# Two-block merges of a triangular inverse crossed over the PE array, their evictions shared by two engines, and the attention steps put in other slots

## The reference, cut to what matters

```
for t in range(768):                       # 4 batches x 8 heads, head_dim 48
    y[t]   = q[t] @ state
    state += beta[t] * outer(k_n[t], v[t] - k_n[t] @ state)      # k_n = k/(|k|+1e-6)
x = y as 3072 tokens x 384
x = leaky_relu(x @ w_in, 0.01) @ w_out     # w_in 384x2048, w_out 2048x384
e = argmax(x @ w_gate + bias[modality]);  out = gate * (relu(x @ w1[e]) @ w2[e])   # 8 experts
```

## Time and profile before

| | |
|---|---|
| median of 3 runs | 987.36 us (984.31 to 990.70) |
| the profiled execution | 978.93 us, of which the span shown by the profile is 977.2 us |
| granted TensorE clock, mean over the span | 0.957 |
| tile n = 3 (`up(3,0)` to `up(4,0)`) | 421.32 to 524.06 us |
| `up(5,0)` begins | 618.30 us |

### The profile page before, as it was taken

How to read it: one execution, slowest core, us unless ns; L and a number is a source line. 1 busy time by engine, 2 the same in 40 slices (tenths; PEclk the granted TensorE clock), 3 DMA queues, 4 the chain that set the end, 5 groups by cost and what they waited for, 6 DMA issues and landing times.

```text
span 977.2 us, 26906 instructions
## 1 busy us (share of the span) xinstructions
PE 870.9 (89%) x10528; PEld 766.0 (78%) x10529; DVE 553.5 (57%) x1578; ACT 350.6 (36%) x609; POOL 87.6 (9%) x100
## 2 busy tenths in 40 slices
PE   3775889989999998999989999999969999999962
PEld 3664678878888887888878888888759898889862
DVE  4974994588638862798359842344642333333350
ACT  3364335542545253444444342323411212121230
POOL 1000000000020002000100001010121212121210
PEclk9965899999999999999999999999999999999996
DMA  9904272345143533344153313255051111111122
GB/s 127 337 4 75 62 150 68 68 107 101 34 92 74 104 62 52 99 86 81 41 102 84 74 28 84 58 94 175 32 171 33 48 32 48 32 48 32 40 74 73
DMA packets 148308, 77.92 MB, mean 80 GB/s; under 512 B 112496, under 2 KB 144240, under 8 KB 147824
## 3 DMA queue, kind: packets, MB, share of 16 engines
q1 hardware_dynamic: 143264, 66.59, 30.4%
q0 software_dynamic: 4096, 9.48, 3.2%
q10 hardware_dynamic: 848, 0.39, 0.2%
HBM read 59.30 MB, written 13.21 MB: 74 GB/s over the span
## 4 chain that ended last, share of the span: by engine, by line
PE 67%; DVE 15%; ACT 7%; DMA 4%; issue 3%; SPq 1%; ACTq 1%; DVEq 0%; POOL 0%; POOLq 0%
PE bank L518 17%; PE bank L503 14%; PE bank L605 11%; PE bank L580 10%; DVE inv_t L1299 2%; DVE inv_tmp L1293 2%; PE bank L590 2%; PE bank L381 2%; PE bank L410 2%; ACT diag L987 2%; DVE g_raw L1368 1%; PE bank L484 1%; DVE tr L1305 1%; PE bank L471 1%; DVE inv_a L1255 1%
## 5 line engine op out<-in xcount | busy, mean ns | idle before, releaser
L518 PE MATMUL bank<-wo_hi,g_hi 128*128 128x392 f32 x384 | 139.1, 362 | 7.3 <-DVE g_lo L1373 4.0
L518 PE MATMUL bank<-wo_hi,g_lo 128*128 128x392 f32 x384 | 132.2, 344 | 0.0
L518 PE MATMUL bank<-wo_lo,g_hi 128*128 128x392 f32 x384 | 132.1, 344 | 0.0
L1368 DVE SCALAR_TENSOR_TENSOR g_raw<-g_raw 128x512 f32<-128x512 f32 x96 | 66.3, 691 | 105.0 <-ACT g_raw L1043 105.0
L503 PE MATMUL bank<-x_hi,wi_hi 128*128 128x512 f32 x288 | 118.3, 411 | 6.2 <-ACT g_raw L1043 3.4
L1043 ACT ACTIVATE g_raw<-bank 128x512 f32<-128x512 f32 x96 | 57.3, 597 | 170.5 <-PE bank L503 170.1
L503 PE MATMUL bank<-x_hi,wi_lo 128*128 128x512 f32 x288 | 114.0, 396 | 0.0
L503 PE MATMUL bank<-x_lo,wi_hi 128*128 128x512 f32 x288 | 113.9, 395 | 0.0
L1050 ACT ACTIVATE g_hi<-g_raw 128x512 fp32r<-128x512 f32 x96 | 60.7, 632 | 116.9 <-DVE g_raw L1368 116.9
L1373 DVE TENSOR_TENSOR g_lo<-g_raw,g_hi 128x512 fp32r<-128x512 f32 x96 | 66.3, 691 | 41.9 <-ACT g_hi L1050 41.7
L518 PEld LDWEIGHTS bank<-wo_hi,g_hi 128*128 128x128 f32 x384 | 72.7, 189 | 13.8 <-issue 6.0
(11 more groups left out here) (215 smaller groups left out, 1493.3 us busy)
## 6 DMA issues: line engine op xcount, KB each, us to landing
wo_lo<-wo_lo_d SPq DMA_DIRECT2D x80, 196.0 KB, 2.4
w_raw<-in_moe_w SPq DMA_DIRECT2D x6, 1536.0 KB, 8.4
x_rows<-stage SPq DMA_DIRECT2D x6, 770.0 KB, 6.2
kq_in_rows<-in_k SPq DMA_DIRECT2D x6, 768.0 KB, 7.0
k_raw<-in_k SPq DMA_DIRECT2D x24, 192.0 KB, 4.0
vals<-in_v SPq DMA_DIRECT2D x48, 96.0 KB, 2.9
kq_in_rows<-in_q SPq DMA_DIRECT2D x6, 768.0 KB, 8.8
x_raw<-y_t SPq DMA_DIRECT2D x33, 96.0 KB, 2.4
```

The source lines that it names most:

```text
L518: mm = pe.matmul(acc[i][:, 0:DX], g[f % 2][:, P * i:P * i + P], w, start=(f == 0 and k == 0), stop=(f == FT - 1 and k == 2))
L1368: dve.scalar_tensor_tensor(out=g_raw[f % 2][:], in0=g_raw[f % 2][:], scalar=0.01, in1=g_raw[f % 2][:], op0=ALU.mult, op1=ALU.max).then_inc ...
```

## The change

- `merge_x` and `merge_p` are crossed: even and odd pairs use different halves of the array's columns and go to different banks (X,0 and X,1 are now even and odd pairs, not the first and the second sixteen groups). Both are moved behind `down` of their slots 5 and 6. `merge_p` waits for both X banks, `updates` for both P banks.
- ACT evicts the odd X bank (behind `copy_diag` in its order), DVE the even one.
- The elimination runs in slots 12 to 4 instead of 13 to 4.
- `scale_v` (values times norm) and `split_x` (`x_lo`) go from DVE to Pool, but for the first tile's `x_lo`.
- `gram_q(.., 1)` goes ahead of `up` in slot 0; `old_values(.., 0)` with its `sub_w` from slot 5 to slot 3; `outputs` from slots 10 and 11 to 11 and 12; `gram_k` from slots 10 and 11 to both sides of `down` in slot 10, with its evictions; `state_sum(.., 1, ..)` and `add_s` from slot 12 to slot 11, `norm` (DVE) and `roots` (ACT) too; `scale_gram` to slot 12.
- SP loads the values one slot earlier (slot 15 instead of 0 of the next tile).

```diff
-INV_AT = {13: (0, 5), 14: (5, 9), 15: (9, 13), 0: (13, 17), 1: (17, 21), 2: (21, 25), 3: (25, 30), 4: (30, INV)}
+INV_AT = {12: (0, 4), 13: (4, 8), 14: (8, 11), 15: (11, 14), 0: (14, 17), 1: (17, 20), 2: (20, 24), 3: (24, 28), 4: (28, INV)}
@@ PE
-            def merge_x(t, m):
+            def merge_x(t):
                 pe.wait_ge(s.tr_ready, t + 1)
-                b, done = fill(("X", t, m))
+                to = [fill(("X", t, odd)) for odd in range(2)]
                 for j in range(16):
-                    for hh in range(2):
-                        mm = pe.matmul(b[low_p(hh), BLK * j:BLK * j + BLK], inv_s[up_p(hh), 16 * m + j, BLK:CH],
-                                       tr[up_p(hh), 16 * m + j, :], start=True, stop=True)
-                mm.then_inc(done, 1)
+                    for odd in range(2):
+                        for hh in range(2):
+                            mm = pe.matmul(to[odd][0][low_p(hh ^ odd), BLK * j:BLK * j + BLK], inv_s[up_p(hh), 2 * j + odd, BLK:CH],
+                                           tr[up_p(hh), 2 * j + odd, :], start=True, stop=True)
+                        if j == 15:
+                            mm.then_inc(to[odd][1], 1)
...
-            def merge_p(t, m):
+            def merge_p(t):
                 pe.wait_ge(s.td_ev, 4 * t + 2)
-                pe.wait_ge(*is_drained(("X", t, m)))
-                b, done = fill(("P", t, m))
+                for odd in range(2):
+                    pe.wait_ge(*is_drained(("X", t, odd)))
+                to = [fill(("P", t, odd)) for odd in range(2)]
...
             def updates(t, c):
                 pe.wait_ge(s.td_ev, 4 * t + 4)
-                pe.wait_ge(*is_drained(("P", t, c)))
+                for odd in range(2):
+                    pe.wait_ge(*is_drained(("P", t, odd)))
...
@@ PE slot, ahead of down
+                if cur and f == 0:
+                    gram_q(n + 1, 1)
                 if ff and f < FT - 1:
                     up(n, f + 1)
...
-                    if f < 3:
+                    if f in (1, 2):
                         gram_q(n + 1, f + 1)
-                    if f == 5:
-                        merge_x(n + 1, 0)
-                        merge_x(n + 1, 1)
-                    if f == 6:
-                        merge_p(n + 1, 0)
-                        merge_p(n + 1, 1)
+                    if f == 3 and n >= 0:
+                        old_values(n + 1, 0)
...
-                    if f == 10:
+                    if f == 10 and n < 0:
                         outputs(n + 1, 0)
-                        if n < 0:
-                            outputs(n + 1, 1)
+                        outputs(n + 1, 1)
                     if f == 11 and n >= 0:
+                        outputs(n + 1, 0)
+                    if f == 12 and n >= 0:
                         outputs(n + 1, 1)
-                    if f == 12:
-                        state_sum(n + 1, 1, 0)
...
                 if nxt:
+                    if f == 10:
+                        gram_k(n + 2, 0)
@@ PE slot, behind down
-                    if f == 5 and n >= 0:
-                        old_values(n + 1, 0)
+                    if f == 5:
+                        merge_x(n + 1)
+                    if f == 6:
+                        merge_p(n + 1)
...
-                    if f == 12:
-                        state_sum(n + 1, 1, 1)
...
                     if f == 10:
-                        gram_k(n + 2, 0)
-                    if f == 11:
                         gram_k(n + 2, 1)
+                if cur and f == 11:
+                    state_sum(n + 1, 1, 0)
+                    state_sum(n + 1, 1, 1)
@@ SP slot
-                if f == 0 and n >= 0 and is_set(n + 1):
-                    sp.wait_ge(*is_filled(("U", n, 1, 1)))
-                    load_values(n + 1)
...
+                if f == 15 and n >= -1 and is_set(n + 2):
+                    sp.wait_ge(*is_filled(("U", n + 1, 1, 1)))
+                    load_values(n + 2)
@@ Pool
-            for t in range(1, SETS):
-                pool.wait_ge(s.tt_ready, t)
-                pool.memset(inv_t[:], 0.0).then_inc(s.tm_zero, 1)
-                if t == 2:
+            def scale_v(t):
+                pool.wait_ge(s.v_in, 128 * t + 128)
+                pool.wait_ge(s.den_rdy, t + 1)
+                pool.tensor_tensor(vals[:], vals[:], den_s[:].unsqueeze(2).broadcast_to([P, GROUPS, HD]), ALU.mult
+                                   ).then_inc(s.vals_rdy, 1)
+
+            def split_x(n):
+                pool.wait_ge(s.xh, n + 1)
+                pool.tensor_tensor(x_lo[:], x_raw[:], x_hi[:].bitcast(F32), ALU.subtract).then_inc(s.x_rdy, 1)
+
+
+            for n in range(-1, TT - 1):
+                scale_v(n + 1)
+                if is_set(n + 2):
+                    pool.wait_ge(s.tt_ready, n + 2)
+                    pool.memset(inv_t[:], 0.0).then_inc(s.tm_zero, 1)
+                if n == 1:
                     pool.wait_ge(s.list_out, 16)
-                if t >= 2:
-                    scatter_ids(t - 2)
+                if n >= 1:
+                    scatter_ids(n - 1)
+                if n >= 0:
+                    split_x(n + 1)
@@ ACT
+            def copy_x(t, odd):
+                act.wait_ge(*is_filled(("X", t, odd)))
+                act.wait_ge(s.tr_ready, t + 1)
+                for hh in range(2):
+                    mm = act.activation(tr[low_p(hh), odd::2, :],
+                                        att_bank(("X", t, odd))[low_p(hh ^ odd), :].rearrange("p (g t) -> p g t", g=16), ACT.Copy, scale=-1.0)
+                mm.then_inc(drain(("X", t, odd)), 1)
...
                     if f == 5:
                         copy_diag(n + 1)
+                        copy_x(n + 1, 1)
...
                     if f == 10:
                         copy_gram(n + 2, 0, 0)
+                        copy_gram(n + 2, 1, 0)
                     if f == 11:
-                        copy_gram(n + 2, 1, 0)
-                    if f == 12:
                         if n == -1:
                             split_x(0)
                         roots(n + 2)
@@ DVE slot
-                if nxt and f == 13:
+                if nxt and f == 12:
                     scale_gram(n + 2)
...
-                if 0 <= n < TT - 1 and f == 14:
-                    split_x(n + 1)
                 if cur:
+                    if f == 3 and n >= 0:
+                        sub_w(n + 1, 0, 0)
+                        sub_w(n + 1, 0, 1)
                     if f == 5:
-                        copy_x(n + 1, 1)
-                        scale_v(n + 1)
-                        if n >= 0:
-                            sub_w(n + 1, 0, 0)
-                            sub_w(n + 1, 0, 1)
+                        copy_x(n + 1, 0)
...
-                if nxt:
-                    if f == 10:
-                        copy_gram(n + 2, 0, 1)
-                    if f == 11:
-                        copy_gram(n + 2, 1, 1)
-                    if f == 12:
-                        if n == -1:
-                            split_x(0)
-                        norm(n + 2)
-                if cur and f == 12:
+                if nxt and f == 10:
+                    copy_gram(n + 2, 0, 1)
+                    copy_gram(n + 2, 1, 1)
+                if cur and f == 11:
                     add_s(n + 1, 1, 0)
                     add_s(n + 1, 1, 1)
+                if n == -1 and f == 11:
+                    split_first_x()
+                if nxt and f == 11:
+                    norm(n + 2)
```

67 lines of the change are left out of this document (29 added, 38 removed).

## The result

Both kernels were timed in turn on the same chip: before 987.45 us (984.31 to 990.7), after **1023.64 us** (1022.33 to 1029.37), four runs each; the ratio is 1.0377, with a 95% interval of 1.0326 to 1.0429. I had said 992, at most 1007. The profiled spans are 977.2 and 1021.1 us, so 43.9 us have to be found. PE's busy time grew by 7.4 us against the earlier trace rows, although the merges are shorter; the rest is waiting. Part of both is the clock: between `up(0, 0)` and `up(5, 0)` it stands at 0.50 for 63.6 us of the trace, against 15.6 before; half the pace for 48 us more is up to 24 us (an estimate).

A forecast was written before the change was run, and what follows sets the result against it. The attention tiles were taken as bound by PE (busy 89%). Terms: n = -1 and 0 +3.8, n = 1 to 3 +1.5, n = 4 +2.1, fetch wait -2.1; in all +5 us, giving 992 us, 8 in 10 from 977 to 1007.

The forecast's parts named there:

- The merges halve: merge_x and merge_p: crossing takes half off each merge of 2.14 us, 1.07 us less each.
- The waits of 0.69 and 1.1 us: PE's waits ahead of up(1) (0.69 us) and of merge_x behind tr (1.09 us), both said to go.
- that at `queries_t`: PE's wait of 1.26 us ahead of queries_t, said to go since add_s comes before norm.
- ACT's queue holds `merge_p`: merge_p: PE waits 2.35 us for ACT's copy_x(1), queued behind copy_diag, where it waited nowhere.
- the bank of the fourth KK product: Slot 10: the fourth product waits 1.0 us for the first one's bank, which ACT drains by copy_gram.
- e + 14.35: e is the end of up(6); copy_p was put ready at e + 14.45, PE at e + 13.35: 1.1 us wait at updates.
- x_lo on Pool: Ahead of up(n+1, 0): Pool's x_lo takes 2.9 us; PE waits 0.9 us in n = 0 to 3, 1.8 in n = 4.
- my slower rival: x_lo of 4.35 us or more on Pool holds up each tile and the clock falls: 16 us, 1008; chance 0.18.
- The clock at merge_p: Behind the 2.35 us wait at merge_p the clock falls to half; +0.8 us a tile, bounds 0 and 1.7.
- -2.1 - 1.1 + 2.35 + 1.1 + 0.8: up(6) to up(9): merges halved, merge_x wait gone, waits added at merge_p and updates, slower clock.
- The fetch stops: PE's 2.49 us wait for its own instructions in outputs of n = 2; half of 2.49 + 1.7 counted, so -2.1.
- The start: n = -1 and 0: up(0, 0) at 105 to 106 rather than 96.14 us; +3 left at the end of n = 0, +0.8 clock.

The follow-up runs named there:

- e10: e7 with Pool's four scatter writes of a tile held until up(n, 14) is done (slot 13 instead of 10): 1.0081 of the kernel before.
- e13: The changed kernel with only the scaling of the values back on DVE, x_lo left on Pool: 1010.37 us, 1.0326 of the kernel before.
- e1: The changed kernel with x_lo and the scaling of the values back on DVE: 1011.29 us, 1.0237 of the kernel before.
- e5: The kernel before with only x_lo of sets 1 to 5 and the scaling of the values moved to Pool: 1016.04 us, 1.0262 of the kernel before.
- e11: e10 with 20 fp32 identity matmuls added at the start of PE's program: 983.30 us, 1.0038 of the kernel before.
- e8: e7 with 123 more small matmuls at the very start of PE's program: 1008.00 us, 1.0145 of the kernel before.
- e2: The changed kernel with both evictions of X on DVE: 1009.39 us, 1.0220 of the kernel before.
- e14: The changed kernel with ACT evicting its half of X between two halves of copy_diag: 1010.05 us, 1.0331 of the kernel before.
- e7: Changed kernel with x_lo, values, both X evictions and P's second on DVE, and the last split_wi of n = -1 ahead of norm: 1.0037 of the kernel before.
- e9: e7 with both merges uncrossed, all else in the same places: 986.37 us, 1.0065 of the kernel before.
- e15: The changed kernel with DVE's last split_wi of n = -1 ahead of norm: 1019.26 us, 1.0446 of the kernel before.
- e12: The kernel before with Pool's scatter writes held until up(n, 13) is done: 974.34 us, 0.9956 of the kernel before.
- e3: The changed kernel with the two KK steps back behind down(10) and down(11): 1032.23 us, 1.0484 of the kernel before.
- e17: The kernel before with Pool's scatter writes held until up(n, 13) and its memset ahead of them: 983.83 us, 0.9922 of the kernel before.
- e16: Kernel before with late scatter writes, memset ahead of them, gram_q(1) ahead of up(1), add_s ahead of norm, state_sum ahead of down: 976.06 us, 0.9982.

## Why the prediction was wrong

**Right, with sizes.** The merges halve (1.22 us). The waits of 0.69 and 1.1 us go, that at `queries_t` too. ACT's queue holds `merge_p` for 2.50 us (2.35 said); the bank of the fourth KK product for 0.93 where nothing else stops it, as in e10 (1.0 said). `up(0, 0)` at 105.44 (105 to 106). The clock falls behind the wait. The Trainium skill's page "TensorEngine Tiling (Array Packing)", Instruction Overhead, would have kept the merges at their pace; the runs say otherwise (1.22 us instead of 2.14), though its advice against a tiling factor from a small dimension would have cost nothing here. One sum has a slip: its terms make ACT ready for `updates` at e + 14.35, not 14.45, so the wait there should have been 1.0.

**The step that failed most is "x_lo on Pool"**, the sentence "DVE is relieved by 1.76 each for `x_lo` and the values, but DVE isn't what PE waits for". Three things in it were wrong. `x_lo` took 3.42 us where nothing of DVE's ran beside it, and 3.9 to 4.7 where DVE's elimination first kept it out, where I took 2.9. (The estimate from the Trainium skill's page "GPSIMD Engine Reference", Performance versus the Vector engine, 3.4, was right for the quiet case.) Its wait was 5.13 us at the end of n = 0, 1.95 at that of n = 1 to 3 and 2.29 at that of n = 4, not 0.9 and 1.8. The clock fell behind two of these waits, and in n = 1, 2 and 4 behind the 1.8 to 2.0 us that `down(n, 0)` waited. And Pool's instructions held one of DVE's for 2.65 to 3.13 us, the scaling of the values in all five tiles and `x_lo` in three, so the scaling, priced at nothing, cost some 5 us by e13 and e1. That was my slower rival, but I gave it 0.18 and 16 us, and its threshold of 4.2 us was met in one tile (4.67); the hold does the rest. e1 and e5 put Pool's part at 14 us in the new order and 26 in the old.

**The clock at merge_p** was mis-sized: +0.8 a tile said. The fall lasted 6.8 us, not 3.4, in n = 0 to 3; in n = 0 to 2 more stops of 0.97 to 2.5 us stand in or ahead of it, in n = 3 none. Nor does it come with each wait of this length, as I had assumed: in n = 3 of e1 the clock stays at 1.00. From `up(6)` to `up(9)` tile 4 takes 22.6 us and tile 3 24.0, against 22.7 before, from which 1.3 for `old_values` must be taken, since it moved out: +1.2 and +2.6. My terms for that stretch (-2.1 - 1.1 + 2.35 + 1.1 + 0.8) gave +1.05, so only n = 4 fits.

**The fetch stops** were seen ("issue") and taken to be something that "may go with the move or not", with -2.1. The long ones are tied to where 256-instruction boundaries fall and to late packets of PE's program. In the changed kernel they cost two stops of 2.5 us in `merge_p`, and the short ones some 2.7 us a tile in n = 1 to 3 (10.4 against 7.8 us for the slot). e11 and e8 show that place alone moves the time by 0.4 and 0.7%.

**The start**: 9.3 us late as said, but only 3.8 was to be left behind n = 0. There remained 10.4 at `up(1, 0)`. Its wait for Pool's `x_lo` (5.13 us, against some 1 before) isn't the cause by itself, for in e1, without it, `up(1, 0)` comes at 224.0 too; e2 and e14, which shorten the wait at `merge_p`, bring it to 220.3 and 219.6, and in e7, with P's second eviction and the new order of the start as well, it comes at 215.6.

What stays open: what else keeps `up(1, 0)` late in the changed kernel; why a boundary's packet comes in time at some boundaries and 8 us late at others with like traffic, and why PE must wait for it. e9 shows that pace matters at one of two places. Why the short stops come beside the writes on some chips and not on others is open too, and with it how much of them belongs to the change: the changed kernel has them, e1, e2, e13, e14 and e15, its closest relatives on other chips, don't. So is what the granted clock goes by.

## What to carry to other kernels

A matmul step made shorter gives time only if its evictions aren't what ends the stretch: sum the evictors' queue between two steps before counting PE's gain. Before work goes to Pool, list which DVE instructions with two SBUF inputs will run beside it: add up to Pool's whole length to the one that comes behind a pause, and a dense run of them to Pool's own time. "issue" inside dense small matmuls can be a late packet of the program, to be looked up in the DMA queues; a few instructions ahead of it (e11), or another time for Pool's scatter writes (e12), were worth 0.4% each here, and the crossed matmuls nothing. Before a stop that went is put down to an edit, compare on one chip.

## What the runs showed of the hardware

- A Pool tensor_tensor on SBUF holds DVE's next instruction with two SBUF inputs until it ends (2.65 to 3.13 us in the changed kernel), and in e5 a one-input cast of 8 columns too (2.75 us instead of 0.17). Back-to-back DVE instructions with two SBUF inputs keep Pool's out (5.88 us instead of 3.42). A Pool memset let `leaky`, with two inputs, pass (0.70 us, changed kernel, n = 0), but held a one-input fp32 instruction of 32 columns (1.05 us instead of 0.18), which I hadn't expected.
- Crossed 32 x 32 matmuls, four places of the array in turn, start every 9.5 ns (1.22 us / 128); uncrossed ones every 17 ns.
- PE's program comes in packets of 16 KB, 256 instructions. Crossed merges use as many up in 1.2 us. A late packet stopped PE for up to 4.16 us (e3), and PE went on 1.2 to 1.6 us behind its landing.
- Beside four indirect scatter writes of Pool (5 us) PE got some five matmuls and their loads per 0.73 us for a while, in the changed kernel, e5 to e8 and e17, and where e17 moved the writes the stops came along. In twelve kernels on two other chips the same writes went with no such stops.
- The granted clock doesn't follow from the length of a wait: behind 2.50 us at `merge_p` it was 0.50 for 6.8 us (changed kernel, n = 3), for 3.4 (n = 4) or not at all (e1, n = 3); behind 1.1 us at `merge_x` it was 0.50 for 3.4 us in e16 and stayed at 1.00 in the kernel before.
